# Folding the last expert's P1 + P6 into P7 once, and storing accumulators as they become final

## The reference

```python
scores = scale * q_c @ k_c^T ; attn = softmax(scores) ; x = attn @ v_c          # (2304, 512)
x = ((x @ w_a) * (x @ w_b)) @ w_out                                             # (2304, 512)
p = domain_probs / (domain_probs.sum(-1, keepdims=True) + 1e-09)
for e in range(4):
    h = np.maximum(x @ w1[e], 0.0)                                              # (2304, 1024)
    out += p[:, e:e + 1] * (h @ w2[e])
```

## Time and profile before

| | us |
|---|---|
| median of 3 runs | 1194.07 (1192.29 to 1195.15) |
| the profiled execution's own time | 1192.56 |
| span of the profile of that execution | 1190.8 |
| TensorE busy | 1172.9 (98% of the span) |
| VectorE busy | 860.6 (72%) |
| ScalarE busy | 502.0 (42%) |

### The profile page before, as it was taken

How to read it: one execution, slowest core, us unless ns; L and a number is a source line. 1 busy time by engine, 2 the same in 40 slices (tenths; PEclk the granted TensorE clock), 3 DMA queues, 4 the chain that set the end, 5 groups by cost and what they waited for, 6 DMA issues and landing times.

```text
span 1190.8 us, 18862 instructions
## 1 busy us (share of the span) xinstructions
PE 1172.9 (98%) x7648; PEld 1131.8 (95%) x7648; DVE 860.6 (72%) x1148; ACT 502.0 (42%) x868; POOL 0.7 (0%) x6
## 2 busy tenths in 40 slices
PE   8999999999999999999999999999999999999997
PEld 7999988899999889999999999999999999999997
DVE  5786879887878883367877777797346677777787
ACT  6555454455445552235444344344233533333332
POOL 0000000000000000000000000000000000000000
PEclk9999999999999999999999999999999999999999
DMA  7296784898777699838777777648894877676761
GB/s 268 95 360 236 283 324 180 319 345 339 301 297 277 261 408 359 316 132 328 299 270 266 279 281 260 244 162 279 254 362 167 339 264 264 248 263 250 263 239 54
DMA packets 73163, 319.56 MB, mean 268 GB/s; under 512 B 7340, under 2 KB 13812, under 8 KB 56692
## 3 DMA queue, kind: packets, MB, share of 16 engines
q1 hardware_dynamic: 73076, 318.35, 72.4%
HBM read 221.81 MB, written 96.51 MB: 267 GB/s over the span
## 4 chain that ended last, share of the span: by engine, by line
PE 88%; DVE 5%; DMA 3%; ACT 2%; issue 1%; SPq 1%; DVEq 0%; ACTq 0%
PE ps L670 29%; PE ps L672 28%; PE ps L671 28%; DMA kept_w<-w 1%; DMA kept_wo<-wo_lone 1%; PE ps L680 1%; PE ps L699 1%; PE ps L707 1%; PE ps L688 1%; DMA kept_w<-lone 1%; DVE wo_three L1640 0%; ACT wo_three L1100 0%; PE ps L743 0%; DVE x L1640 0%; SPq L453 0%
## 5 line engine op out<-in xcount | busy, mean ns | idle before, releaser
L670 PE MATMUL ps<-x,wab 128*128 128x384 f32 x504 | 169.3, 336 | 0.6 <-ACT ps L1100 0.5
L672 PE MATMUL ps<-x,wab 128*128 128x384 f32 x504 | 168.4, 334 | 0.0
L671 PE MATMUL ps<-x,wab 128*128 128x384 f32 x504 | 168.4, 334 | 0.0
L1100 ACT ACTIVATE hw<-xraw 128x768 fp32r<-128x768 f32 x112 | 94.9, 847 | 163.3 <-DVE xraw L2116 80.7
L1100 ACT ACTIVATE ps<-ps 128x384 f32<-128x384 f32 (+1 forms) x184 | 91.5, 502 | 162.8 <-PE ps L672 159.9
L670 PE MATMUL ps<-hw,w2s 128*128 128x384 f32 x448 | 151.6, 338 | 0.0
L670 PE MATMUL ps<-x,w1s 128*128 128x384 f32 x448 | 151.5, 338 | 0.0
L672 PE MATMUL ps<-x,w1s 128*128 128x384 f32 x448 | 149.8, 334 | 0.0
L672 PE MATMUL ps<-hw,w2s 128*128 128x384 f32 x448 | 149.8, 334 | 0.0
L671 PE MATMUL ps<-hw,w2s 128*128 128x384 f32 x448 | 149.7, 334 | 0.0
L671 PE MATMUL ps<-x,w1s 128*128 128x384 f32 x448 | 149.7, 334 | 0.0
(11 more groups left out here) (198 smaller groups left out, 2262.8 us busy)
## 6 DMA issues: line engine op xcount, KB each, us to landing
wab<-kept_ab SPq DMA_DIRECT2D x70, 512.0 KB, 4.7
w1s<-kept_w SPq DMA_DIRECT2D x32, 1024.0 KB, 6.3
w2s<-kept_w SPq DMA_DIRECT2D x16, 2048.0 KB, 7.5
w1s<-kept_w SPq DMA_DIRECT2D x16, 1536.0 KB, 6.1
w2s<-kept_w SPq DMA_DIRECT2D x16, 1536.0 KB, 6.3
kept_ab<-wab SPq DMA_DIRECT2D x42, 512.0 KB, 5.4
raw<-in_w SPq DMA_DIRECT2D x16, 1024.0 KB, 10.6
kept_w<-w SPq DMA_DIRECT2D x16, 1024.0 KB, 13.0
```

The costliest lines, as they stand in the source:

```text
L670: pe.matmul(dst, stat(HI), mov(HI), start=first, stop=False, skip_group_check=True)
L671: pe.matmul(dst, stat(HI), mov(LO), start=False, stop=False, skip_group_check=True)
L672: return pe.matmul(dst, stat(LO), mov(HI), start=False, stop=last, skip_group_check=True)
L1100: return act.activation(dst, src, ACT.Copy)
```

## The change

ScalarE gets one more instruction, its last: a copy of U (banks 2 and 3) into `c2[:, GU]`, which is free once the folding is done. It raises `u_part`. VectorE then forms P7 + U once, in `c2[:, G7]`, and adds this sum to G4 and to G5, and U to G53, from SBUF. The two additions of P7 alone and the three of U from PSUM are gone: five instructions become four. G4's addition now raises the third count of `evac` ("a7") and G5's the fourth ("u"), and the store of G4 waits for the third.

```diff
 # sync engine
                 if T == NTH - 1:
-                    for name, n in (("u", G4), ("u", G5), ("c11", G11)):
+                    for name, n in (("a7", G4), ("u", G5), ("c11", G11)):
                         sp.wait_ge(evac, evac_no(T, PH - 1, name))
 # scalar engine, end of a window
                 hi(S4, H11)
+                if T == NTH - 1 and w == PH - 1:
+                    act.wait_ge(o6_made, 2 * V + 2)
+                    act.wait_ge(folded, 4 + 4)
+                    copy(c2[:, GU], block_of(2)).then_inc(u_part, 1)
 # vector engine
                 def add_a7():
                     dve.wait_ge(o7_made, 2 * V + 2)
-                    if not final:
-                        add_to(c2[:, G7], 6, "a7").then_inc(evac, 1)
-                    else:
-                        dve.wait_ge(evac, evac_no(T, w, "a5"))
-                        dve.tensor_tensor(acc_t[:, G4], block_of(6), acc_t[:, G4], ALU.add).then_inc(folded, 1)
-                        dve.tensor_tensor(acc_t[:, G5], block_of(6), acc_t[:, G5], ALU.add).then_inc(evac, 1)
+                    add_to(c2[:, G7], 6, "a7").then_inc(evac, 1)
 ...
                     add_a5()
-                    add_a7()
+                    if not final:
+                        add_a7()
 ...
                 else:
-                    dve.tensor_tensor(acc_t[:, G53], block_of(2), acc_t[:, G53], ALU.add).then_inc(folded, 1)
+                    dve.wait_ge(u_part, 1)
+                    dve.tensor_tensor(c2[:, G7], block_of(6), c2[:, GU], ALU.add).then_inc(folded, 1)
                     dve.wait_ge(folded, 4 + 5)
-                    dve.tensor_tensor(acc_t[:, G4], block_of(2), acc_t[:, G4], ALU.add).then_inc(u_part, 1)
-                    dve.wait_ge(evac, evac_no(T, w, "a7"))
-                    dve.wait_ge(u_part, 1)
-                    dve.tensor_tensor(acc_t[:, G5], block_of(2), acc_t[:, G5], ALU.add).then_inc(evac, 1)
+                    dve.wait_ge(evac, evac_no(T, w, "a5"))
+                    dve.tensor_tensor(acc_t[:, G4], acc_t[:, G4], c2[:, G7], ALU.add).then_inc(evac, 1)
+                    dve.tensor_tensor(acc_t[:, G5], acc_t[:, G5], c2[:, G7], ALU.add).then_inc(evac, 1)
+                    dve.tensor_tensor(acc_t[:, G53], acc_t[:, G53], c2[:, GU], ALU.add).then_inc(folded, 1)
                 dve.wait_ge(o2_made, 2 * V + 2)
                 add_to(acc_t[:, G11], 0, "c11").then_inc(evac, 1)
```

## The result

Eleven executions of the changed kernel had a median of 1189.52 us (1188.02 to 1193.38), eleven of the kernel before 1194.42. The ratio is 0.9964, with a 95% interval from 0.9948 to 0.998. By that ratio the kernel became faster by 4.3 us, where the forecast had 2.2. In both the change gains. How much of the gain belongs to the tail, the profile shows.

What follows compares the result with a forecast made beforehand. The prediction took a backlog of five stores, 4.18 us of traffic, to set the end. 2.00 us (two blocks leaving it) plus 0.19 (G11's store earlier) gave 2.19, from 1194.07 to 1191.9 us, range 1189.9 to 1193.9.

Steps and rivals of the forecast that it cites:

- VectorE's steps: Tail additions: five become four, 0.87 us from start to start, 1.05 if dependent; VectorE ends 1.05 us earlier.
- (a): Stores at the end: their traffic backlog sets the end; gain 2.19 us (1.9 to 2.4), chance 0.62.
- The split of the sum: Tail gain: 2.00 us from two blocks leaving the backlog plus 0.19 from G11's store issued earlier, together 2.19 us.
- (b): Last stores: SyncE's issuing sets the end, half stores keep 0.947 us each; gain 1.05 to 1.67 us, chance 0.20.
- (e): Ahead of P7 + U: ScalarE's copy comes late; each us past 1180.1 costs one us; slower, chance 0.04.
- What the Trainium skill has for a DMA: Last stores: a DMA takes 2.0 us plus its bytes at 436 GB/s, 2.45 us for a half store.
- The time: Whole kernel: median predicted at 1191.9 us, range 1189.9 to 1193.9; three runs before lay 1.8 below to 1.1 above median.
- within 0.2%: Whole kernel: measured change under 2.39 us, not told from no change; chance 0.56, against faster 0.40 and slower 0.04.
- Anything before 1177 us has moved: Ahead of the tail: a shift of more than a few tenths of a microsecond would show the prediction wrong.

Runs made afterwards that it cites:

- order_only: The kernel before with its five PSUM additions reordered, G4's store released behind its own addition, no ScalarE copy; ratio 0.9991, tail 10.14 us against 11.53.
- sum_late: The changed kernel with G53's addition first and the stores of G4 and G5 both waiting for G5's addition; ratio 0.999, tail 10.27 us.
- less_before: The kernel before without the last part's stores of G4 and G5; tail 10.41 us against 11.53.
- less_after: The changed kernel without the last part's stores of G4 and G5; tail 9.28 us against 9.24.
- copy_twice: The changed kernel with ScalarE copying U once more, into a scratch tile, ahead of the copy VectorE waits for; tail 9.72 us against 9.24.
- g11_first: The changed kernel with G11's addition ahead of G53's addition of U; median 1189.96 us, ratio 0.9975, tail 8.85 us.
- after_again: The changed kernel run once more, unaltered, in a second set; median 1192.26 us of 12, ratio 0.9985, tail 9.23 us.
- warm_after: The changed kernel with 40 extra matmuls in TensorE's idle stretch at 157 us; median 1189.73 us, ratio 0.9963, tail 9.23 us.
- warm_before: The kernel before with 40 extra matmuls in TensorE's idle stretch at 157 us; median 1191.62 us, ratio 0.9988, tail 11.53 us.

## Why the prediction came out as it did

The mechanism held, and the steps came out within 0.13 us of the forecast. How the prediction shares the gain out between the steps did not hold. On the scale of the trace before (the times above less 1.76):

| step | forecast | measured |
|---|---|---|
| ScalarE's copy starts, ends | 1179.06, 1179.87 | 1178.97, 1179.79 |
| P7 + U starts | 1180.13 | 1180.12 |
| G4's addition starts | 1181.18 | 1181.11 |
| G4's store issued | 1182.22 | 1182.15 |
| G11's addition starts | 1183.79 | 1183.72 |
| bytes of G11 start | 1185.66 | 1185.53 |
| last bytes | 1187.84 | 1187.74 |
| end of the span | 1188.59 | 1188.50 |

- *VectorE's steps.* Right but for the dependent step behind L2220, which took 0.99 us, not 1.05. The additions from SBUF start 0.87 us apart, as those from PSUM did. The shorter time that the Trainium skill gives to SBUF operands (VectorE: DVE Perf Modes, "The TRN2 errata") does not show in these rows either.
- *The traffic sets the end, (a).* Right: unbroken from G11 on, for 2.21 us where I had 2.18. The gap ahead of G11 was 0.43 us, not 0.6: G4 and G5 took 2.11 us, not 2.00, and G11's bytes started 0.13 earlier. The tail's gain of 2.29 us lies in the 1.9 to 2.4 of (a). order_only and sum_late came out as the same account says.
- *The split of the sum.* The prediction gives 2.00 us to the two blocks that leave the backlog and says that of VectorE's 1.05 only 0.19 counts. As an account of where bytes lie in time this adds up, but as an account of causes it is wrong. Without those blocks the kernel before gains only 1.12 us (less_before), since G11's store then waits for VectorE. The other 1.13 us (less_before to less_after) are VectorE's earlier end, which counts in full. order_only agrees: the blocks leave the backlog, G11's addition starts only 0.20 us earlier (1189.00 - 1183.61 = 5.39 against 5.59), and the gain is 1.39.
- *SyncE's issues, (b).* This rival fell: the half stores' issues took 0.35 to 0.40 us. The prediction's reason against it, that they had the most stores ahead, is borne out by less_before.
- *The copy late, (e).* It did not happen, but copy_twice shows that its price was stated rightly.
- *What the Trainium skill has for a DMA* (DMA: Bandwidth & Descriptors, "Anatomy of one DMA"), 2.45 us for a half store, looks met by the 2.4 to 2.5 us measured from issue to landing after the change, but those half stores still stood behind G11. In g11_first, with hardly any wait behind G11, they took 1.9 to 2.0. For a whole block the same rule, which is fitted on another issuing path, gives an estimate of 2.90 us, and the trace has 2.3 where the queue was empty. So on SyncE's queue it is 0.5 to 0.6 us too long, and the 3.0 to 3.5 of before held 1.1 us of queueing or more. That is more than the prediction's figures suggest.
- *The time.* Median 1189.52 in the first set, 1192.26 in the second. The first lies 0.4 us under the low end of the range (1189.9), the second in it. The step that was mis-sized is the scatter. I took it from three runs, 2.9 us wide, and 74 executions of the kernel before now spread over 8.3 us (1190.16 to 1198.47). That the likeliest outcome was "within 0.2%" rested on 2.19 against 2.39 us; the two sets gave 4.3 and 1.8, one on either side of that line, and the pooled 2.8 is nearer to "faster". That the second median lies so near to the forecast of 1191.9 is luck as much as insight: half of the executions of one kernel spread over 3 us.
- *"Anything before 1177 us has moved".* It had, by 1.76 us, so this sign of a wrong prediction appeared. It was badly chosen: the code ahead of 1177 us is unchanged, and 1.34 us of the shift come from a stretch at half the clock whose length differs from execution to execution.

What stays open: where the remaining 0.5 us between the pooled 2.8 and the tail's 2.29 lies. It is half of the interval, so it may be nothing. Whether the clock's fall at 13 to 28 us can be avoided was not tried.

## What to carry to other kernels

When results are stored at the end, work back from the last byte. Stores that can be released while the last additions still run cost nothing (less_after: the tail without them is no shorter). What counts is when the last unbroken run of traffic can start, which an engine's addition may set, and how long it is; so finish and release whole blocks one by one, and merge additions that several blocks share. A shift of 0.2% must be read from the same stretch in two traces, from one fixed instruction on: here that gave 2.29 or 2.30 us for each of the three profiles of the change (after, after_again, warm_after) while whole times moved by 8 us.

## What was not expected of the hardware

- A store's issue by SyncE takes 0.33 to 0.47 us while few stores are in flight, and 0.94 to 0.95 behind three whole blocks that were issued within 1.4 us (before, warm_before, sum_late). Behind three that were issued over 3 us it took 0.33 to 0.37 (g11_first).
- TensorE's idle 2.7 us at 157 us is followed by half the clock in some executions and not in others with the same idle time: after_again idled for 2.91 us there and g11_first for 3.32, and both kept the full clock to their last matmul. The Trainium skill (TensorE: Matmul & The Clock Gate, "Part 1: The HAM clock gate") has idleness bring the clock down and activity bring it back; the six profiles agree in that the fall follows the idle time, and three show that idleness of this length need not bring it.
- The end costs about 0.8 us between the last byte and the last instruction (0.75 and 0.76 as the stretches above are cut). Read to 0.01 us it is 0.80 to 0.82 us in all twelve profiles, whatever the traffic ahead of it.
